# Attention, MoE and FFN in one kernel: the FFN takes its rows in order of expert, and the attention's rows are turned by transposes

## The reference

```python
batch, n_heads, seq, head_dim = (4, 8, 768, 64)          # 3072 tokens, 512 features
state = gamma * state + k[:, :, t] (outer) v[:, :, t]
y[:, :, t] = scale * q[:, :, t] @ state
# MoE, E = 8, F = 1024
logits = x @ w_gate;  e_idx = argmax(logits)
gate_w = softmax(logits)[e_idx];  eom = sigmoid(x @ w_output_gate)
out[mask] = gate_w[mask] * eom[mask, e] * (relu(x[mask] @ w1[e]) @ w2[e])
# FFN, 2048 wide
h = x @ w_in;  out = (h - tanh(h)) @ w_out
```

## Time and profile before

| | |
|---|---|
| median of 3 runs | 1056.47 us (1053.91 to 1057.15) |
| the profiled execution, its own time | 1055.47 us |
| its span, first to last instruction | 1053.6 us |
| PE busy | 1017.4 us (97%) |
| DVE, ACT, POOL busy | 667.4, 300.6, 367.6 us |
| mean granted clock of PE | 0.992 of full speed |

### The profile page before, as it was taken

How to read it: one execution, slowest core, us unless ns; L and a number is a source line. 1 busy time by engine, 2 the same in 40 slices (tenths; PEclk the granted TensorE clock), 3 DMA queues, 4 the chain that set the end, 5 groups by cost and what they waited for, 6 DMA issues and landing times.

```text
span 1053.6 us, 18553 instructions
## 1 busy us (share of the span) xinstructions
PE 1017.4 (97%) x5744; PEld 843.0 (80%) x5745; DVE 667.4 (63%) x1270; ACT 300.6 (29%) x540; POOL 367.6 (35%) x325
## 2 busy tenths in 40 slices
PE   8999887999999999998899999999999999999998
PEld 7878766888888888886678878887887887888887
DVE  4766746444343434433687878868877787877775
ACT  1212122222222222221133333333333333333333
POOL 4587696659567858716500000000000000000000
PEclk9999998999999999999899999999999999999999
DMA  9999677677786877835000010010001001000001
GB/s 352 330 339 332 216 233 242 220 233 249 229 269 223 274 247 243 276 135 178 9 21 11 11 50 20 10 40 20 13 7 50 20 10 49 11 0 22 18 1 40
DMA packets 70969, 138.37 MB, mean 131 GB/s; under 512 B 7056, under 2 KB 39184, under 8 KB 70928
## 3 DMA queue, kind: packets, MB, share of 16 engines
q1 hardware_dynamic: 21888, 73.41, 20.7%
q10 hardware_dynamic: 45200, 51.82, 15.2%
q0 software_dynamic: 3840, 12.59, 3.6%
HBM read 98.73 MB, written 39.06 MB: 131 GB/s over the span
## 4 chain that ended last, share of the span: by engine, by line
PE 80%; POOL 8%; issue 6%; DVE 4%; DMA 1%; ACT 1%; ACTq 0%; POOLq 0%; DVEq 0%
PE banks L1148 18%; PE banks L1150 18%; PE banks L1149 18%; PE banks L1240 8%; PE banks L1242 8%; PE banks L1241 8%; POOL w_sb L383 3%; POOL v_scaled L417 2%; POOL w_sb L379 2%; POOL x_sorted L404 1%; PE banks L1219 1%; DMA q_step_sb<-in_q_step 1%; PE banks L1085 1%; DVE tanh_sb L981 1%; PE banks L1074 1%
## 5 line engine op out<-in xcount | busy, mean ns | idle before, releaser
L383 POOL TENSOR_TENSOR w_sb<-raw,w_sb 128x1024 fp32r<-128x1024 f32 x80 | 191.5, 2394 | 6.7
L1240 PE MATMUL banks<-x2T_hi,w_sb 128*128 (+1 forms) x384 | 152.8, 398 | 4.8 <-DVE g_sb L983 4.8
L396 POOL DMA_INDIRECT gathered<-y_sorted,row_back x20 | 22.4, 1121 | 374.5 <-DVE x_sb L948 373.9
L1242 PE MATMUL banks<-x2T_lo,w_sb 128*128 (+1 forms) x384 | 150.5, 392 | 0.0
L1241 PE MATMUL banks<-x2T_hi,w_sb 128*128 (+1 forms) x384 | 150.2, 391 | 0.0
L1150 PE MATMUL banks<-w_sb,g_hi 128*128 128x512 f32 x384 | 149.4, 389 | 0.0
L1148 PE MATMUL banks<-w_sb,g_lo 128*128 128x512 f32 x384 | 149.4, 389 | 0.0
L1149 PE MATMUL banks<-w_sb,g_hi 128*128 128x512 f32 x384 | 149.4, 389 | 0.0
L890 DVE TENSOR_TENSOR hidT_lo<-banks,hidT_hi 128x512 fp32r<-128x512 f32 x62 | 40.0, 686 | 143.6 <-ACT hidT_hi L576 143.5
L637 ACT ACTIVATE square<-banks 128x512 f32<-128x512 f32 x96 | 57.4, 598 | 195.2 <-PE banks L1242 195.2
L1148 PE MATMUL banks<-w_sb,hidT_lo 128*128 x248 | 98.0, 395 | 10.3 <-POOL w_sb L383 5.9
(11 more groups left out here) (129 smaller groups left out, 1662.5 us busy)
## 6 DMA issues: line engine op xcount, KB each, us to landing
raw<-in_weights SPq DMA_DIRECT2D x80, 512.0 KB
in_sb<-in_rows SPq DMA_DIRECT2D x48, 512.0 KB
hid_rows<-hid ACTq DMA_DIRECT2D x31, 512.0 KB, 3.3
hid_quads<-hid_rows ACTq DMA_DIRECT2D x31, 512.0 KB, 4.3
xs_sb<-x_sorted ACTq DMA_DIRECT2D x124, 64.0 KB, 3.1
y_sorted<-ys_sb ACTq DMA_DIRECT2D x31, 256.0 KB, 3.2
out_rows<-out_sb SPq DMA_DIRECT2D x24, 256.0 KB, 2.2
x_sorted<-zeros ACTq DMA_DIRECT2D x1, 2048.0 KB, 23.6
```

The source lines that it names most:

```text
L383: nc.gpsimd.tensor_tensor(w_sb[:, s, 1, lo:hi], raw[:, p % RAW_SLOTS], w_sb[:, s, 0, lo:hi].bitcast(fp32), ALU.subtract).then_inc(piece_do ...
L1240: T.matmul(out_, w_lo, hi, start=first, stop=False)
L1242: return T.matmul(out_, w_hi, lo, start=False, stop=last)
```

## The change

1. The FFN runs over the rows as the experts left them. `y_sorted` has one row for each token without gaps (3072 + 128): `store_rows` stores at a row read from a table (`store_row`, four more DVE instructions after the first `x_lo`). `compact_rows` (in place of `rows_before` and `rows_after`) finds each token's place; POOL writes a table `row_table` of (token, scale) with 24 indirect transfers of 128 entries of 8 bytes (`store_table`), between the splits of the third and the fourth expert. `compact_rows` and `token_scales` now stand together in DVE's fourth step.
2. FFN tile j needs only the first 4j + 12 tiles of the MoE, so its rows are loaded by plain transfers (`load_sorted`, 8 each): the first tile's by ACT in MoE step 25, the others by SP.
3. ACT scales the rows (`x2_scale`, four instructions of 128 columns per subtile), DVE transposes blocks (`x2_turn`), and PE's 24 groups of transposes are gone. The first tile's are done in MoE steps 26 to 30.
4. `up(0,0)`, `up(0,1)` and `up(0,2)` stand between and behind the last two `rows_out`; all `stay_warm` of the FFN is gone.
5. The FFN's rows leave by 24 indirect transfers of POOL (`store_sums`) in place of SP's stores.
6. Attention: the logits are four matmuls of 16 columns summed in PSUM, the rows four transposes of 128 columns (`is_transpose` form), each kind into a bank of its own; DVE copies 16 columns.
7. SP loads six pieces beside the attention (every third chunk) and not eight; the other two are split after the tables are made.
8. Smaller: `load_rows` stands behind `load_hidden` in ACT's step; `hidden(1)` has banks of its own; `rows_out` writes bank 7; more steps of ACT's and DVE's MoE loops are written out.

```diff
-PIECE_LOADED_AT = [CHUNKS + 2 * n for n in range(2 * RAW_SLOTS)]
+PIECE_LOADED_AT = [CHUNKS + 3 * n for n in range(SET_PIECES - 2)]
...
+            def store_table(t):
                 pool.indirect_dma_start(
+                    out=row_table, out_offset=bass.IndirectOffsetOnAxis(ap=compact_row[:, t:t + 1], axis=0),
+                    in_=token_table[:, t].bitcast(i32), in_offset=None,
+                ).then_inc(table_stored, 16)
...
+            for p in range(EARLY_PIECES, SET_PIECES):
+                split_piece(0, 0, p)
             split_pieces(0, 1)
+            for n in range(2, EXPERTS + 1):
+                before = pool.value_load(tiles_through[0:1, n - 2:n - 1], min_val=1, max_val=MOE_TILES)
+                split_pieces(n // 2, n % 2, before)
+                if n == 2:
+                    pool.wait_ge(table_made, 1)
+                    for t in range(TOKEN_TILES):
+                        store_table(t)
...
+            def x2_scale(j, m, first=False):
+                for s in range(m, ROWS_EACH, SUBTILES):
+                    scaled = nc.scalar.activation(rows[:, s], rows[:, s], ACT.Copy, scale=scales[:, s, 1:2])
...
+                if number == 3:
+                    compact_rows()
+                    token_scales()
...
+                V.transpose(x2_bank(m, first).rearrange("p (k b g) -> p g k b", k=DK, g=QUADS),
+                            rows.rearrange("p g (k a) -> p g k a", k=DK)).then_inc(x2T_done, 1)
...
                 for k in range(DK):
-                    last = T.matmul(x_parts[:, k], xT_sb[:, k], ident_gates_sb[:, k], start=True, stop=True)
+                    last = T.matmul(logits, xT_sb[:, k], gates_sb[:, k], start=k == 0, stop=k == DK - 1)
+                last.then_inc(logits_summed, 1)
+                if not first:
+                    pe.wait_ge(x_copied, t)
+                for k in range(DK):
+                    last = T.transpose(x_rows[:, k * P:(k + 1) * P], xT_sb[:, k], ident[:])
                 last.then_inc(x_done, 1)
...
-            stay_warm(WARM_FFN[0], ident)
-            for m in range(SUBTILES):
-                transpose_x2(0, m, first=True)
-            for c in range(LAG):
-                stay_warm(WARM_FFN[c + 1], ident)
-                up(0, c)
-            stay_warm(WARM_FFN[LAG + 1], ident)
+            up(0, 0)
+            rows_out(MOE_TILES - 2, MOE_TILES, (MOE_TILES - 2) % 2)
+            up(0, 1)
+            rows_out(MOE_TILES - 1, MOE_TILES + 1, (MOE_TILES - 1) % 2)
+            up(0, 2)
             with pe.Fori(0, FFN_TILES - 1) as j:
                 for c in range(FFN_CHUNKS):
-                    if c + LAG in X2_SPLIT_AT:
-                        transpose_x2(j + 1, X2_SPLIT_AT.index(c + LAG))
                     up(j, c + LAG)
                     down(j, c)
```

More of the change, by code:

```diff
@@ L109, in build_program @@
     a = Region(slot1_at, rest_at)
+    ident = a.place("ident", [P, P])
     q_decay_sb = a.place("q_decay_sb", [P, CHUNKS, D])
@@ L305, in build_program, with hid_banks, x2_bank, tiles_before @@
         TWO = 2
+        def hid_banks(number):
+            return (at(4), at(5)) if number == 1 else (at(1), at(2))
+        def x2_bank(m, first):
+            return at((4 if first else 6) + m % 2)
+        def tiles_before(j):
+            return min(MOE_TILES, SUBTILES * j + SUBTILES + EXPERTS)
+        def load_sorted(engine, j, rows, scales, ready):
+            tile_rows = slice(j * WIDE, (j + 1) * WIDE)
+            for quad in range(QUADS):
+                part, cols = slice(quad * QUAD, (quad + 1) * QUAD), slice(quad * (D // QUADS), (quad + 1) * (D // QUADS))
+                engine.dma_start(rows[part], y_sorted[tile_rows, cols].rearrange("(b s) c -> b s c", s=ROWS_EACH)).then_inc(ready, 16)
+                engine.dma_start(scales[part].rearrange("b s x -> b (s x)").bitcast(i32),
+                                 row_table[tile_rows].rearrange("(b s) x -> b (s x)", s=ROWS_EACH)).then_inc(ready, 16)
         @block.sync
@@ L487, in copy_state, with copy_x @@
                   .then_inc(state_copied, 1)
-            def copy_x(b, c, first=False, last=False):
+            def copy_x(b, c, first=False):
                 t = b * CHUNKS + c
@@ L678, in tile @@
                     copy_sums(j)
-            with act.Fori(0, FFN_TILES - 1) as j:
+            tile(0, range(LAG, LAG + FFN_CHUNKS), first=True)
+            with act.Fori(1, FFN_TILES - 1) as j:
                 tile(j, range(LAG, LAG + FFN_CHUNKS))
@@ L1161, in hidden @@
                 pe.wait_ge(xsT_lo_done, i + 1)
-                if not first:
+                if number == 2:
+                    pe.wait_ge(relu_done, 2)
+                elif number > 2:
                     pe.wait_ge(relu_done, i * 2)
```

405 lines of the change are left out of this document (200 added, 205 removed).

## The result

The changed kernel takes 1066.7 us (median of four runs, 1063.0 to 1070.6) against 1056.2 beside it: a ratio of 1.0107 (95% interval 1.0076 to 1.0139). It is 1.1% slower, and 38 us above the upper end of the forecast range. Its profiled execution took 1063.4 us with a span of 1061.5, against 1053.6 before.

A forecast was written before the change was run, and what follows sets the result against it. PE, busy 97% of the span, was taken to bound the kernel. The terms -25.6 - 2.4 - 14.0 + 3.1 - 5 + 0 = -43.9 gave 1011.6, as a median 1013 us, range 1001 to 1029.

The forecast's parts named there:

- The table of 24 transfers: POOL's table writes ahead of weight set 3: 1.29 us an issue, nothing lost up to 1.5 us, cost 0.
- (a): Rival: table transfers hold POOL longer; at 2.2 us each PE waits 17 us for set 3, 1030 us; chance 0.11.
- (b): Rival: table transfers above 3.3 us each eat the whole gain ahead of `hidden(11)`; at 3.6, 1063 us; chance 0.03.
- Passage: From MoE to FFN: the 25.6 us loss goes, 0 to 4 may remain; two result-bank hand-over gaps go, -2.4.
- Rival (e): Passage to the FFN: a wait of 5 to 12 us between last `rows_out`s and `up`s, 1018 to 1025; chance 0.08.
- Start of the MoE: First `hidden` to end of `rows_out(2)`: copy moved ahead of the small-instruction chain gains -5 us, bounds -9 and -1.
- The lump: Thirteen small DVE instructions together ahead of tile 2's transposes and second copy, needed by `rows_out(2)`: 11 us (7 to 14).
- Attention: Logits and row transposes per chunk: 1.2 us against 1.18, so no change; at most -7 us, at worst +4.
- the dear end: Attention's upper estimate per chunk: logit passes and transposes each 0.11 us apart, 1.32 us together.
- FFN: Five FFN tiles: 2.8 us each of PE transposes and waits go, -14.0 us, between -14 and 0.
- End: After the last matmul: four POOL stores issued 1.29 us apart, landing 3.9 us after issue; +3.1 us, bounds +1 and +5.

The follow-up runs named there:

- run 13: Changed kernel with ACT's queue reordered, DVE's small routing instructions dealt out, table writes in three bursts of eight, attention of before: 1023.6 us, ratio 0.9686.
- run 2: Changed kernel with the table's 24 indirect transfers replaced by one direct transfer on POOL, order by expert left out: 1046.3 us, ratio 0.9912.
- run 5: Changed kernel with one move undone, ACT issuing row loads ahead of `hid_hi` again: 1052.3 us, ratio 0.9972.
- run 9: Kernel before the change with only the attention's part of the change added: 1060.1 us, ratio 1.0056.
- Versions 1 to 8: Kernels of the first eight follow-up experiments, each the changed kernel with one or several edits; from 1069.6 us down to 1030.4 us.
- run 6: Changed kernel with the same burst of 24 transfers, each 8-byte entry in a 512-byte row of its own: 1069.6 us, ratio 1.012.
- run 15: Changed kernel with ACT's and DVE's MoE loops beginning at step 5 instead of 9: 1065.6 us, ratio 1.0096.
- run 12: Changed kernel with queues mended and small routing instructions dealt out (1030.4), table writes now in three bursts of eight behind sets 3, 4 and 5: 1025.7 us.

## Why the prediction was wrong, step by step

The span grew by 7.9 us where -43.9 was forecast. The step that failed first is the price of the table: I took a row of 24 transfers for free because POOL had time for it, and it cost PE 18.3 us. Then come step 25 of ACT (13.3, priced at nothing, and enlarged by a move that I had counted as a gain), the FFN (7.6), the attention (5.0), the end (3.5) and the start of the MoE (1.5). Some 2.6 us of the 51.8 are left within the MoE and the passage, as many as in run 13, and are not traced.

**The table of 24 transfers** (0 cost up to 1.5 us an issue). The measured 1.26 us met the condition, no wait for set 3 came, and the term failed by 18 us in the trace and 20 by run 2. I had asked how long each transfer holds POOL, and not what 24 of them in a row do to the others. The trace of before has four gathers in a row and two more straight behind them, at 496.83 and 498.33; I extended this fourfold without a bound. Rivals (a) and (b) had the right culprit with the wrong price, the issue.

**Passage** (-25.6 - 2.4). Right in mechanism: with the causes gone, run 13 gains 25.4 of the 28.0 us (the rest lies within the 0 to 4 left open), and in the changed kernel PE had one wait of 1.0 us between 475 and 525. Missing was the way there: eight transfers on ACT at step 25, priced at nothing, and DVE's `x2_turn` ahead of the copy. Rival (e) had a wait of this size (10.4 us, 13 with the clock), but at another place, between the last `rows_out`s, so it did not foresee this one.

**Start of the MoE** (-5). Measured from the first `hidden` to the end of `rows_out(2)`: 57.7 to 54.2, -3.5, inside the bounds. The lump was there. But "`load_rows` no longer holds up `hid_hi`" had the sign wrong: the move delays the store of each result by some 4 us, a step that I had not followed beyond the engine's next instruction (run 5, 14 us).

**Attention** (0, bounds -7 to +4). Measured +5.0 after, about +6 alone (run 9), beyond the bound. The eight logit passes were the dear end as taken (0.91 for 0.88). The transposes took 0.14 us each, not the 0.11 that I had worked out from the length of a row. Above all I took 1.2 where the nearest rows gave 1.32, and held that transfers would cover what goes beyond. They did not: DMA share fell from the 0.99 of the earlier trace rows to 0.88 while PE was full.

```profile
20.00:60.00 40.00, 39.98 (x617) 34.19 (x617) 26.43 (x98) 8.06 (x16) 19.67 (x19) 1.00 0.88 309
```

PE had been the bound already. The rule of the Trainium skill that I weighed there ("TensorE: Matmul & The Clock Gate", "LDWEIGHTS (loading the stationary operand)"), 107 ns for a load of 128 columns, gave 2.4 us for the part. Run 9 agrees with it for the logits (114 ns a pass), and it was nearer than my value.

**FFN** (-14.0). A steady tile lasts 886.14 - 798.63 = 87.51 us (first store of two tiles, POOL's timeline), against 89.82 before and 87.04 predicted: -11.6.

```profile
798.63 1.48 POOL L427 DMA_INDIRECT out_rows<-out_sb,sorted_ids  x1 [82.28 <-ACT out_sb L693]
...
886.14 1.48 POOL L427 DMA_INDIRECT out_rows<-out_sb,sorted_ids  x1 [82.23 <-ACT out_sb L693]
```

The other 5.2 us are lost outside the steady tiles, 3.4 of them in two waits at the start of tile 0 (PE, and the DVE instruction in question):

```profile
536.77 0.50 PE L1274 MATMUL banks<-x2T,w_sb 128*128 x1 [1.91 <-DVE g_sb L1015]
...
545.61 0.50 PE L1274 MATMUL banks<-x2T,w_sb 128*128 x1 [1.50 <-DVE g_sb L1015]
```

```profile
533.37 1.99 DVE L1020 TENSOR_TENSOR g_lo<-g_sb,g_hi 128x512 fp32r<-128x512 f32 x1
```

That subtraction took 0.69 us a step earlier; at 542.15 it takes 2.05. POOL splits the last four weight pieces beside it until 543.7. It is what the earlier trace rows showed at the start of the MoE; I had not applied it to the new place where DVE's chunks and POOL's pieces meet. Versions 1 to 8 have both waits too, in two of them the second at 3.1 us.

**End** (+3.1, bounds 1 to 5). Measured +6.6. The fourth store is issued 3.0 us after the last matmul's start, as worked out (row below). The span ends 7.2 us after that; I had taken 3.9, from a gather. The landing is given as 2.7 us after issue; what fills the rest was not tried.

```profile
1054.31 0.96 POOL L427 DMA_INDIRECT out_rows<-out_sb,sorted_ids  x1 [0.30 <-issue]
```

In run 13, as stages: +0.6 - 30.9 - 6.5 + 6.5 = -30.3 us of span, against -43.9. What is left of the miss there is the FFN (7.5 us: its start, and tiles 0.5 us longer than forecast), the end (3.4), and the 2.6 us above.

## What to carry to other kernels

When a change puts many transfers of one queue in a row, the time on the issuing engine is not their price: a row longer than any in the trace has no bound from it, and breaking it up cost nothing here (24 in a row: 18 us; three times eight: nothing found). When an instruction moves on a queue, follow the loop that goes through that queue round to its start. Here some 4 us more between a copy and its store showed as no wait in most steps and cost 14 us. And where two resources are both nearly full, find out which one bounds before you call added work covered.

## What the runs showed of the chip

- A row of 24 indirect transfers 1.26 us apart, 128 entries each: after 13 us with PE at full rate, its matmuls come up to 2.8 us apart, ACT stands with its operand ready, the DMA engines are nearly idle (share 0.02), until some 4 us after the last issue. It needs no shared line (run 6), it comes with ACT and DVE in code already run (run 15), and eight in a row behind the next set don't bring it on (run 12). What the engines wait for is not shown. Holding the number in flight down by waits was not tried. The Trainium skill ("DMA: Bandwidth & Descriptors", "SWDGE vs HWDGE vs iDMA") says that POOL's transfers get descriptors written by software into rings in SBUF, with one context for all; no run here tells whether the rings have a part in it.
- Matmuls of 16 columns with 128 weight columns start 0.114 us apart, those of 144 columns 0.147.
- A DVE subtraction of 512 columns with two inputs in SBUF takes 0.69 us alone and 1.99 to 2.05 beside POOL's split of a weight piece.
